# First exponential ahead of the copy, divisors behind the maxima, and one mask at a time for the transposes: sparse attention in a fused attention and mixture-of-experts kernel

## The reference

```
# q, k, v: 4 batches x 8 heads x 576 tokens x 64, tau = 0.02
scores = scale * (q @ k.T)
thresh = max(scores, axis=-1) - tau
scores = where(scores >= thresh, scores, -1e9)
attn = exp(scores - max(scores))
attn = attn / (sum(attn) + 1e-9)
x = attn @ v                       # 2304 tokens x 512
# then: x = moe(x)    8 experts, one expert per token, 512 -> 1024 -> 512
# then: out = moe2(x) 4 experts, each applied to every token, weighted
```

## Time and profile before

| what | us |
|---|---|
| median of three runs | 1481.06 |
| the profiled execution | 1480.6 |
| span of its instructions | 1478.8 |
| TensorE busy in the span | 1428.0 |
| VectorE busy | 733.0 |
| ScalarE busy | 572.0 |
| GpSimd busy | 152.9 |
| mean granted TensorE clock | 0.987 |

### The profile page before, as it was taken

How to read it: one execution, slowest core, us unless ns; L and a number is a source line. 1 busy time by engine, 2 the same in 40 slices (tenths; PEclk the granted TensorE clock), 3 DMA queues, 4 the chain that set the end, 5 groups by cost and what they waited for, 6 DMA issues and landing times.

```text
span 1478.8 us, 27432 instructions
## 1 busy us (share of the span) xinstructions
PE 1428.0 (97%) x10398; PEld 1248.2 (84%) x10398; DVE 733.0 (50%) x1174; ACT 572.0 (39%) x1016; POOL 152.9 (10%) x302
## 2 busy tenths in 40 slices
PE   7999999993899999999999999999999999999999
PEld 5777777762788888899999999999989999999998
DVE  5777777767677777765222243222332222432222
ACT  5666776661566665654111122121221111311111
POOL 2222222210111112211000000000000000000000
PEclk9999999995999999999999999999999999999999
DMA  4322222203788888885000011000020000100001
GB/s 84 68 64 62 61 63 65 50 18 92 230 286 271 275 270 291 294 281 190 0 1 0 1 59 56 1 0 1 27 88 1 1 0 1 58 22 22 22 22 43
DMA packets 156075, 127.26 MB, mean 86 GB/s; under 512 B 88768, under 2 KB 129824, under 8 KB 156000
## 3 DMA queue, kind: packets, MB, share of 16 engines
q1 hardware_dynamic: 148304, 103.94, 23.4%
q0 software_dynamic: 6640, 21.97, 4.1%
q10 hardware_dynamic: 1056, 0.26, 0.1%
HBM read 110.02 MB, written 16.12 MB: 85 GB/s over the span
## 4 chain that ended last, share of the span: by engine, by line
PE 89%; DVE 4%; ACT 2%; DMA 2%; issue 2%; SPq 1%; DVEq 0%; ACTq 0%
PE front L824 9%; PE front L826 9%; PE front L825 9%; PE front L811 6%; PE back L811 6%; PE back L813 6%; PE back L812 6%; PE front L813 5%; PE front L812 5%; PE back L612 5%; PE back L825 3%; PE back L826 3%; PE back L824 3%; PE front L637 3%; PE front L655 3%; DVE pr L1128 2%
## 5 line engine op out<-in xcount | busy, mean ns | idle before, releaser
L991 ACT ACTIVATE hth<-front 128x384 fp32r<-128x384 f32 (+1 forms) x132 | 61.0, 462 | 508.1 <-PE front L813 506.9
L824 PE MATMUL front<-wh,hth 128*128 128x512 f32 x584 | 229.4, 393 | 1.6 <-DVE htl L1324 1.6
L826 PE MATMUL front<-wh,htl 128*128 128x512 f32 x584 | 227.7, 390 | 0.0
L825 PE MATMUL front<-wl,hth 128*128 128x512 f32 x584 | 227.6, 390 | 0.0
L1296 DVE TENSOR_TENSOR wl<-ring,wh 128x1024 fp32r<-128x1024 f32 x160 | 191.6, 1222 | 54.5 <-ACT wh L982 52.8
L982 ACT CAST wh<-ring 128x1024 fp32r<-128x1024 f32 x160 | 163.7, 1053 | 76.3 <-DMA ring<-in_moe_w 76.0
L811 PE MATMUL front<-xch,wh 128*128 128x384 f32 (+1 forms) x528 | 170.4, 323 | 4.4 <-DVE xcl L1304 4.3
L813 PE MATMUL front<-xch,wl 128*128 128x384 f32 (+1 forms) x528 | 169.9, 322 | 0.0
L812 PE MATMUL front<-xcl,wh 128*128 128x384 f32 (+1 forms) x528 | 169.8, 322 | 0.0
L811 PE MATMUL back<-xch,wh 128*128 128x384 f32 (+1 forms) x528 | 169.1, 320 | 0.6 <-DVE htl L1310 0.6
L813 PE MATMUL back<-xch,wl 128*128 128x384 f32 (+1 forms) x528 | 169.0, 320 | 0.0
(11 more groups left out here) (225 smaller groups left out, 2511.0 us busy)
## 6 DMA issues: line engine op xcount, KB each, us to landing
ring<-in_moe_w SPq DMA_DIRECT2D x160, 512.0 KB, 4.0
tokens_x<-x_nat SPq DMA_DIRECT2D x16, 288.0 KB, 4.5
x_nat<-compact_y POOLq DMA_DIRECT2D x6, 768.0 KB, 7.0
raw<-in_q SPq DMA_DIRECT2D x32, 128.0 KB, 2.5
vv<-in_v SPq DMA_DIRECT2D x32, 128.0 KB, 2.2
raw<-in_k SPq DMA_DIRECT2D x30, 128.0 KB, 2.6
vv<-in_v SPq DMA_DIRECT2D x64, 16.0 KB, 2.1
out<-x_nat SPq DMA_DIRECT2D x3, 256.0 KB, 2.1
```

The costliest lines, as they stand in the source:

```text
L824: pe.matmul(acc_bank[t], hth[:, f, ts], w2_block(wh, f), start=f == 0, stop=False)
L825: pe.matmul(acc_bank[t], hth[:, f, ts], w2_block(wl, f), start=False, stop=False)
L826: last = pe.matmul(acc_bank[t], htl[:, f, ts], w2_block(wh, f), start=False, stop=f == KF - 1)
L991: act.activation(hth[:, f, 0:n], hb(f, n), ACT.Relu).then_inc(s_hh, 1)
```

## The change

It has three parts.

1. ScalarE: in each step the first exponential is issued before the wait for the transposes and the copy of the first four turned blocks, and not behind them. The order is then exponential, copy, exponential, copy.
2. VectorE: at `i` = 2 the two operations on the divisors stand between the maxima and the masks, and no longer behind the masks.
3. TensorE: `turn` is split. The first four transposes wait for the first mask alone, and the other five for the second (at `i` = 0, where the step before has one tile, the one wait stays). The wait for the bank of the second four (`s_eb`, or `s_kd` at `i` = 1) goes with the second part.

```diff
@@ tensor
-                    pe.wait_ge(s_prob, done)
+                    pe.wait_ge(s_prob, done if i == 0 else done - 1)
+                    turn_first((j - 1) % US, far_main(j + 1))
+                    if i != 0:
+                        pe.wait_ge(s_prob, done)
                     if i != 0 and not (zero_h and j < 2):
                         if i == 1:
                             if not last_unit(last, bp):
...
-                    turn((j - 1) % US, far_main(j + 1), near(j + 1))
+                    turn_rest((j - 1) % US, near(j + 1))
@@ scalar
-                if not (zero_h and j < 1):
-                    act.wait_ge(s_ta, n)
-                    evacuate((j - 1) % US, 0, far_main(j + 1)).then_inc(s_ea, 1)
                 for t in range(tiles_in(j)):
                     act.wait_ge(s_nmax, done + t + 1)
                     if not (zero_h and x + t < 2):
                         act.wait_ge(s_prob, done + t - 1)
                     act.activation(ex[(x + t) % 2][:], whole(j, t), ACT.Exp, bias=nmax[:, x + t:x + t + 1]).then_inc(s_exp, 1)
+                    if t == 0 and not (zero_h and j < 1):
+                        act.wait_ge(s_ta, n)
+                        evacuate((j - 1) % US, 0, far_main(j + 1)).then_inc(s_ea, 1)
@@ vector
                     dve.tensor_reduce(nmax[:, x + t:x + t + 1], whole(j, t), AX.X, ALU.max, negate=True).then_inc(s_nmax, 1)
+                if i == 2 and not (zero_h and bp == 0):
+                    divisors(h if bp == 1 else h - 1, 1 - bp)
...
-                if i == 2 and not (zero_h and bp == 0):
-                    divisors(h if bp == 1 else h - 1, 1 - bp)
```

More of the change, by code:

```diff
@@ L642, in scores, with turn_first, turn_rest @@
                 pe.matmul(g[:, 512:512 + P], q1, b[hi, k0 + FB:k0 + SEQ], start=True, stop=True).then_inc(s_scores, 1)
-            def turn(j, main, to):
-                buf = pr[j % 2]
-                if tiles_in(j) == 1:
-                    for kb in range(4):
[L649 to L660, removed]
+            def turn_first(j, main):
+                first = own_blocks(j, 0)
+                for kb in range(4):
+                    last = pe.transpose(main[:, kb * P:(kb + 1) * P], pr[j % 2][:, (first + kb) * P:(first + kb + 1) * P], ident[:])
+                last.then_inc(s_ta, 1)
+            def turn_rest(j, to):
+                second = own_blocks(j, 1)
+                if tiles_in(j) == 2:
+                    for kb in range(4):
+                        last = pe.transpose(TURN[:, kb * P:(kb + 1) * P], pr[j % 2][:, (second + kb) * P:(second + kb + 1) * P], ident[:])
+                    last.then_inc(s_tb, 1)
+                pe.transpose(blk(to), pr[j % 2][:, 4 * P:5 * P], ident[:]).then_inc(s_tc, 1)
             def last_unit(last, bp):
@@ L724, in _ @@
             pe.wait_ge(s_prob, UT * HEADS)
-            turn(US - 1, far_main(US + 1), near(US + 1))
+            turn_first(US - 1, far_main(US + 1))
+            turn_rest(US - 1, near(US + 1))
             pe.wait_ge(s_ea, US * HEADS)
```

## The result

Five runs of the changed kernel gave a median of 1472.63 us (1471.98 to 1473.29), five of the kernel before 1480.56 us. The ratio is 0.9947, with a 95% interval of 0.9932 to 0.9962: 7.9 us faster. The prediction was 1474.1 us from a median of 1481.06, a gain of 7.0 us.

The account below looks back on a forecast made before the run. TensorE bounds attention, stalled by masks once per unit. Loop -4.5, other units -1.4, register operations -1.5, end +0.4 make -7.0 us: 1474.1 us from 1481.06, within 1.2 us (chance 0.45); 1472.2 to 1478.4 at eight in ten.

Parts of the forecast that it names:

- The stall of 0.62 us at i = 2: TensorE in attention waits for VectorE's masks once per unit; 16 units make about 9.9 us, nearly all attention can give.
- Part 1 makes the scores of i = 2 wait for the copy: ScalarE's later copy delays TensorE's scores, so step i = 1 grows by 0.23 us in 15 or 16 units.
- The cover in the other steps: In other two-tile steps the later copy takes 3.34 us against a 3.69 us step, leaving 0.3 us of room.
- Without a stall at i = 2: TensorE's transposes start earlier, gaining 0.38 us per unit: 4.5 us in 12 loop units, 1.4 us in four outside.
- The register operations: Moving them from between scores and transposes on TensorE gains 0.06 us in 24 steps, 1.5 us with the other units.
- The first rival: TensorE's pipe empties between the two groups of four transposes, 0.18 us in 64 steps: 1487.1 us, chance 0.07.
- The divisors: At i = 2 on VectorE, ScalarE's exponential hides them in their new place: no cost, at most 0.33 us x 15.
- The end of attention: In the last step the copies move behind the exponential and TensorE waits for them: 0.4 us lost once.
- The sum: Whole kernel: -4.5 - 1.4 - 1.5 + 0.4 = -7.0 us, giving a predicted time of 1474.1 us.
- The Trainium skill's sequencer loop: Queued transposes on TensorE would fully hide the two register operations, making the gain 0.08 and not 0.06 us per step.

Follow-up runs that it names:

- e1: Kernel before with only the split of the transposes, copy ahead of both exponentials and divisors behind the masks as before; 1472.67 us, ratio 0.9946.
- e2: Kernel before with only ScalarE's first exponential moved ahead of the copy; 1479.36 us, ratio 0.9996.
- x2: Changed kernel with two more register operations and two satisfied waits ahead of the first group of transposes, in 24 loop steps; 1471.72 us, ratio 0.9942.
- e3: Kernel before with only the divisors moved between maxima and masks; 1480.34 us, ratio 1.0000.
- e4: Changed kernel with the divisors back behind the masks; 1473.42 us, ratio 0.9951.
- e8: Changed kernel with the bank wait ahead of the second group's mask wait, and the copy ahead of the exponential in attention's last step; 1472.82 us, ratio 0.9947.
- x1: Changed kernel with two more register operations and two satisfied waits between the two groups of four transposes, in 24 loop steps; 1472.49 us, ratio 0.9951.
- e7: Changed kernel with the second group of transposes waiting for the bank first, then for the second mask; 1472.44 us, ratio 0.9947.

## Why the prediction was right, and where not

- *The stall of 0.62 us at i = 2, once per unit, and nothing else to gain.* Right. Steps i = 0 and 4 didn't move, and i = 2 is at its pace within 0.03 us. "Nothing else" holds but for 0.07 us at i = 1 and at i = 3, of which more below.
- *Part 1 makes the scores of i = 2 wait for the copy, +0.23 us at i = 1.* Right to the hundredth: 3.34 us, with 0.23 us of idle time ahead of L637. The cover in the other steps held, and no other scores of the loop wait. Against the pace that the split alone gives step i = 1, 3.04 us, the copy costs 0.30 us.
- *Without a stall at i = 2, 0.38 us per unit, 4.5 us in the loop.* The path is right: the second mask ends at 202.55 and is covered by the first four transposes. The prediction gave the gain to the two parts together; e1 and e2 show that the split brings all of it. The earlier exponential moves the same wait from the first mask (e1) to the copy (changed kernel): 6.97 against 6.99 us for the two steps.
- *The register operations, 1.5 us.* The size was nearly met (against the 3.69 us of before, 0.07 us at i = 3 and 0.04 us at i = 2, which is 1.3 us in 12 units), by luck: the change removes the very wait that I had read as the cost of instructions. The cause was wrong. What left step i = 3 was the wait of all nine transposes for the second mask, which ended 0.13 to 0.14 us before them. e2 takes it away with the register operations in place, and x2 puts two more of them there at no cost. The first rival's 0.18 us had the same fault: it set the 0.28 us against the 0.10 us inside the scores, but 0.20 us is the plain distance from scores to transposes (e2 at i = 3). I had taken the difference of two gaps as the price of instructions, without asking when the mask for which they waited had ended. The waits view didn't list it.
- *The divisors, nothing.* Right, in both directions (e3, e4).
- *The end of attention, 0.4 us lost.* Right: 8.55 against 8.15 us, and back to 8.07 where the copy goes first (e8).
- *The sum.* -7.0 us predicted, -7.3 in the profiles and -7.9 in the medians. The loop gave -5.8 (5.9 predicted with the register term), head 0 and the part of head 7 before its last step -1.9 (1.5 predicted). The rest of the difference to the medians is within what the runs scatter.
- *The Trainium skill's sequencer loop* (Advanced Engine Details and Errata, Sequencer Loop): engine instructions go into a queue, and others can be read and queued while a control instruction executes. By that, work already queued covers a register operation. x1 and x2 agree, with 0.00 us for two register operations and two satisfied waits in 12 steps, and for one wait of its own in 12 others. The prediction counted 0.06 us in each of 24 steps for such operations. Had I held to the rule in both places, the 0.28 us gap would have asked for another cause.

## What to carry to other kernels

Where a group of operations waits for several inputs and needs them one after the other, give each its own wait: the work on the first covers the lateness of the second. Moving a producer forward on a busy engine moves its neighbour back (here the copy, for which the next scores wait); do the split first and see whether the move still buys anything. Before a gap is priced as the cost of the instructions in it, compare its end with the end of every input that it waits for.

## What the runs showed of the hardware

- A product whose wait for a VectorE mask came last started 0.05 us behind the mask (L641 in e1: 201.81 to 201.86); with that wait on a register operation and another behind it, it was 0.13 us (L655 in e2: 206.88 to 207.01). The weight loads of L656 show the same pair: 0.05 us in e7 (202.34 to 202.39) and 0.12 us in the changed kernel (202.55 to 202.67).
- Two register operations with two satisfied waits cost TensorE nothing measurable, between two groups of transposes (x1) or between scores and transposes (x2): step i = 2 of pair 0 stays at 3.65 us and i = 3 at 3.62 us.
- The stages behind attention took between 1160.9 and 1164.3 us in these profiles. Two profiles of the same changed kernel differ there by 2.1 us (1163.1 and 1160.9), and by 0.05 us in where attention ends (308.40 and 308.35).
